# Second expert layer in pairs of 256 tokens, its first product as three fp32r products

## The reference, cut to what matters

```python
logits = x @ w_gate                      # 512 x 8
e_idx = np.argmax(logits, axis=1)        # one expert for each token
gate_w = softmax(logits)[arange, e_idx]
eom = 1.0 / (1.0 + np.exp(-(x @ w_output_gate)))
for e in range(8):
    mask = e_idx == e
    h = np.maximum(x[mask] @ w1[e], 0.0)             # 512 x 1024
    out[mask] = gate_w[mask] * eom[mask, e] * (h @ w2[e])   # 1024 x 512
```

## Time and profile before

| | |
|---|---|
| median of 3 runs | 690.13 us (688.09 to 690.76) |
| profiled execution, device time | 688.13 us |
| its span | 686.4 us |
| PE busy | 658.4 us, 96% |
| DVE, ACT, POOL busy | 60%, 49%, 43% |
| mean granted TensorE clock | 0.998 |

### The profile page before, as it was taken

One profiled execution on the slowest core, in us unless ns is written; L12 is line 12 of the kernel. 1 busy time (PEld: TensorE's weight loads), 2 busy tenths in 40 slices (PEclk: granted clock), 3 DMA queues, 4 the chain that ended last, 5 costly groups with the idle time before them and its releaser, 6 DMA issues.

```text
span 686.4 us, 15791 instructions
## 1 busy us (share of the span) xinstructions
PE 658.4 (96%) x5939; PEld 564.5 (82%) x5949; DVE 409.9 (60%) x859; ACT 337.0 (49%) x507; POOL 295.2 (43%) x287
## 2 busy tenths in 40 slices
PE   8989999999999989899999999989999999999995
PEld 5569889888888876479998998547999999999894
DVE  7878888788888857755454635375245254443421
ACT  4568999999999886331334312232213213231200
POOL 4357999989999871021221322002132132122121
PEclk9999999999999999999999999999999999999999
DMA  9301231111220439748489964654545654941000
GB/s 279 94 2 47 55 86 49 47 48 48 60 82 25 143 129 334 280 131 310 160 301 349 349 241 142 233 208 130 192 160 173 248 174 172 372 176 51 19 31 32
DMA packets 45988, 105.77 MB, mean 154 GB/s; under 512 B 5459, under 2 KB 11603, under 8 KB 45936
## 3 DMA queue, kind: packets, MB, share of 16 engines
q1 hardware_dynamic: 38464, 87.65, 36.8%
q0 software_dynamic: 4544, 12.70, 5.8%
q10 hardware_dynamic: 2928, 4.72, 2.0%
HBM read 87.64 MB, written 13.11 MB: 147 GB/s over the span
## 4 chain that ended last, share of the span: by engine, by line
PE 53%; DVE 3%; DMA 2%; issue 1%; ACT 0%; POOL 0%; POOLq 0%; ACTq 0%; DVEq 0%
PE hT_ps_layer L1381 27%; PE y_ps_layer L1394 7%; PE y_ps_layer L1398 7%; PE y_ps_layer L1401 7%; PE x_turn_layer L1368 2%; DMA x<-x_mid 1%; PE hT_ps_layer L1310 1%; PE hT_ps_layer L1308 1%; PE x_turn_layer L1298 1%; DVE row_one_hot_layer L1210 1%; DMA x_tile_layer<-x_src,token_to_read_layer 1%; PE hT_ps_layer L1323 1%; DMA x_mid<-y_out_layer,y_token_layer 0%; PE count_ps_layer L1298 0%; PE rank_ps_layer L1298 0%
## 5 line engine op out<-in xcount | busy, mean ns | idle before, releaser
L1381 PEld LDWEIGHTS hT_ps_layer<-xT_layer,w 128*128 128x128 f32 x1664 | 189.6, 192 | 3.8 <-DVE xT_layer L1243 1.7
L1381 PE MATMUL hT_ps_layer<-xT_layer,w 128*128 128x128 f32 x1664 | 190.2, 275 | 0.8 <-issue 0.8
L438 POOL TENSOR_TENSOR probs_lo<-probs,probs_hi 128x768 f16<-128x768 f32 x89 | 146.1, 1649 | 33.0 <-ACT probs_hi L353 30.4
L1132 ACT ACTIVATE hT_hi_layer<-hT_ps_layer 128x512 fp32r<-128x512 f32 x52 | 31.1, 597 | 239.2 <-PE hT_ps_layer L1381 239.2
L565 DVE TENSOR_REDUCE max_halves<-turn 128x1 f32<-128x384 f32 x180 | 94.7, 553 | 31.8 <-PE turn L729 30.2
L1270 DVE SCALAR_TENSOR_TENSOR hT_lo_layer<-hT_ps_layer,hT_hi_layer 128x512 fp32r<-128x512 f32 x52 | 34.6, 689 | 88.0 <-ACT hT_hi_layer L1132 77.0
L345 ACT ACTIVATE probs<-scores 128x768 f32<-128x768 f32 x96 | 79.9, 832 | 11.3 <-PE scores L753 10.3
L1445 POOL DMA_INDIRECT out_dram<-y_out_layer,y_token_layer x16 | 19.7, 1234 | 147.1 <-DVE y_out_layer L1281 147.1
L353 ACT ACTIVATE probs_hi<-scores 128x768 f16<-128x768 f32 x96 | 80.2, 836 | 1.2 <-PE pv L777 0.9
L1127 ACT ACTIVATE w_hi<-w 128x1024 fp32r<-128x1024 f32 x64 | 62.4, 1047 | 26.6 <-issue 26.6
L1250 DVE TENSOR_TENSOR w_lo<-w,w_hi 128x1024 fp32r<-128x1024 f32 x64 | 74.0, 1219 | 0.0
(11 more groups left out here) (227 smaller groups left out, 1087.5 us busy)
## 6 DMA issues: line engine op xcount, KB each, us to landing
w<-in_moe_w_dram SPq DMA_DIRECT2D x32, 2048.0 KB, 11.2
w<-in_v_dram ACTq DMA_DIRECT2D x4, 768.0 KB, 7.1
qk_raw<-in_q_dram SPq DMA_DIRECT2D x16, 192.0 KB, 3.2
qk_raw<-in_k_dram SPq DMA_DIRECT2D x16, 192.0 KB, 3.5
qB<-qA SPq DMA_DIRECT2D x16, 192.0 KB, 2.7
kB<-kA SPq DMA_DIRECT2D x16, 192.0 KB, 3.1
x_src<-x SPq DMA_DIRECT2D x2, 1536.0 KB, 17.0
x_mid<-x SPq DMA_DIRECT2D x2, 1536.0 KB, 18.3
```

The lines of the kernel that those rows point to most:

```text
L438: nc.gpsimd.tensor_tensor(p_lo[slot][:], probs[slot][:], p_hi[slot][:], ALU.subtract).then_inc(p_lo_pool, 1)
L1381: t = nc.tensor.matmul(hp[n][:, i * P:(i + 1) * P], W1[par][:, c, f * P:(f + 1) * P], xT[:, c, :], start=(c == 0), stop=(c == CD - 1))
```

## The change

In the second layer only:

- A step is a pair of tiles, 256 tokens of one expert. The table counts pairs; `read_tok` and the like have 30 columns instead of 24. An expert's last pair may be half or nearly empty, and is computed in full.
- The first product is three fp32r products of 256 moving columns: W1H x xTH, W1H x xTL, W1L x xTH. W1H and W1L lie in one buffer each (the place of `W2H[1]` and of the old `W2L`), so W2H has one buffer now and W2L a new one. DVE makes W1H by a copy and W1L by a subtraction, after the last pair of the expert before; for the first expert ACT and DVE make them at the end of layer one.
- x is gathered straight into the buffer that PE turns, two gathers for a pair; the `stage` copies and `turn_in` go. ACT takes the high part of the turned x, DVE the low part.
- ACT makes the output from PSUM (there are two banks for it), with the gate as a scale; DVE no longer does.
- The first product has four PSUM banks of two chunks each.

`w1_split(e)` is what DVE does after the last pair of expert e, for expert e + 1. The core of the diff, engine by engine:

```diff
         @blk.tensor
-            turn_x(0)
-            warm(5)
...
+            def turn_pair(g):
+                pe.wait_ge(x_in, 32 * g + 32)
+                for c in range(CD):
+                    for u in range(2):
+                        at = (c % 2) * R + u * P
+                        t = nc.tensor.transpose(tp[c // 2][:, at:at + P], xin[:, u, c * P:(c + 1) * P], ident[:])
+                    if c % 2 == 1:
+                        t.then_inc(x_turned, 1)
+
+            def pair_body(g, pair, par):
+                e = 2 * pair + par
+                pe.wait_ge(x_lo, 2 * g + 2)
+                for f in range(CF):
+                    b, i = divmod(f, 2)
+                    if i == 0:
+                        pe.wait_ge(w1_lo, W1_STEPS * e + f * W1_STEPS // CF + 1)
+                    h_ps = hp4[b][:, i * R:(i + 1) * R]
+                    at = slice(f * P, (f + 1) * P)
+                    for c in range(CD):
+                        nc.tensor.matmul(h_ps, W1H[:, c, at], xTH[:, c, :], start=(c == 0), stop=False)
+                        nc.tensor.matmul(h_ps, W1H[:, c, at], xTL[:, c, :], start=False, stop=False)
+                        t = nc.tensor.matmul(h_ps, W1L[:, c, at], xTH[:, c, :], start=False, stop=(c == CD - 1))
+                    if i == 1:
+                        t.then_inc(h_bank, 1)
+                turn_pair(g + 1)
+                for u in range(2):
+                    pe.wait_ge(y_ready, 2 * g + u + 1)
+                    at = slice(u * P, (u + 1) * P)
+                    for b in range(4):
+                        if u == 0:
+                            pe.wait_ge(h_hi, 4 * g + b + 1)
+                        for f in (2 * b, 2 * b + 1):
+                            nc.tensor.matmul(yp2[u][:], hH[:, f, at], W2H[par][:, f, :], start=(f == 0), stop=False)
+                        if u == 0:
+                            pe.wait_ge(w2_lo, W2_STEPS * e + b + 1)
...
+                    t.then_inc(y_done, 1)
...
         @blk.scalar
+            def x_to_hi(g):
+                for b in range(2):
+                    act.wait_ge(x_turned, 2 * g + b + 1)
+                    nc.scalar.activation(xTH[:, 2 * b:2 * b + 2, :].rearrange("p c n -> p (c n)"), tp[b][:], ACT.Copy).then_inc(x_hi, 1)
+
+            def pair_body(g, pair, par):
+                for b in range(4):
+                    act.wait_ge(h_bank, 4 * g + b + 1)
+                    nc.scalar.activation(hH[:, 2 * b:2 * b + 2, :].rearrange("p c n -> p (c n)"), hp4[b][:], ACT.Relu).then_inc(h_hi, 1)
+                x_to_hi(g + 1)
+                act.wait_ge(y_free, g + 1)
+                for u in range(2):
+                    act.wait_ge(y_done, 2 * g + u + 1)
+                    nc.scalar.activation(yout[:, u, :], yp2[u][:], ACT.Copy, scale=gate_col[:, u:u + 1]).then_inc(y_ready, 1)
...
         @blk.vector
+            def pair_body(g, pair, par):
+                for b in range(4):
+                    dve.wait_ge(h_hi, 4 * g + b + 1)
...
+                x_to_lo(g + 1)
...
+            def w1_split(e, pair, par):
+                if isinstance(e, int) and e == E - 1:
+                    return
+                dve.wait_ge(w1_ready[1 - par], 16 * (pair + par + 1 + E // 2))
+                for i in range(W1_STEPS):
+                    c = slice(i * F // W1_STEPS, (i + 1) * F // W1_STEPS)
+                    nc.vector.tensor_copy(W1H[:, :, c], W1[1 - par][:, :, c]).then_inc(w1_hi, 1)
+                    if i > 0:
+                        w1_rest(e + 1, 1 - par, i - 1)
+                w1_rest(e + 1, 1 - par, W1_STEPS - 1)
+                w1_taken(e + 1)
+                split(e + 1, None, 1 - par)
...
         @blk.gpsimd
+            def pair_body(g, pair, par):
+                pool.wait_ge(x_turned, 2 * g + 4)
+                nc.gpsimd.tensor_copy(gid[:], cols_of(read_tok, 2 * g + 4)).then_inc(gid_ready, 1)
...
+                gather_pair(gid)
+                pool.wait_ge(y_sent, 32 * g + 16)
+                nc.gpsimd.tensor_copy(gate_col[:], cols_of(gate_of, 2 * g)).then_inc(y_free, 1)
...
         @blk.scalar
...
             if first:
+                act.wait_ge(w1_ready[0], 16 * (1 + E // 2))
+                act.wait_ge(weights_over, 1)
+                for i in range(W1_STEPS - 1):
+                    c = slice(i * F // W1_STEPS, (i + 1) * F // W1_STEPS)
+                    nc.scalar.activation(W1H[:, :, c], W1[0][:, :, c], ACT.Copy).then_inc(w1_hi, 1)
```

## The result

Five runs of the changed kernel have a median of 693.57 us (692.69 to 694.40), five of the kernel before 690.56 (688.09 to 690.76): 1.0054 times as long, 95% interval 1.0035 to 1.0072. The medians lie 3.0 us apart, and the interval of the ratio is 2.4 to 5.0 us slower. The profiled execution took 692.69 us with a span of 691.0; before it was 688.13 and 686.4.

What follows compares the result with a forecast made beforehand. PE's own work was taken as the bound. 3.7 + 2.8 - 0.15 gave +6.3 us on the 686.4 span: 692.7, or 694.4 for the device; counted from 689.1, 695.5 us. Range: 686 to 703.

Steps and rivals of the forecast that it cites:

- the nine pairs: Layer two's loop on PE: nine pairs of 23.65 us, 212.9 against 209.2 for sixteen tiles, +3.7 us.
- between the layers: End of layer one: making expert 0's W1H and W1L there costed at nothing, up to 1 us if layer two starts late.
- a spacing below 119.4 ns: First-product matmul starts: 122 to 123 ns apart expected; below 119.4 the time is within 0.5%, below 111.3 faster.
- 15.9 ns over the columns: First product: surplus for each fp32r matmul, taken from the second product, giving 122.6 ns each, 11.77 us a pair.
- the surplus stands once for each matmul: fp32r matmuls: time over columns / 2.4 does not grow with the columns; 15 to 22 ns in the readings used.
- Rivals 1 and 2: First product 111.6 or 108.4 ns a matmul, 686 or 683, chance 0.19; surplus 4.9 in both products, 681, chance 0.08.
- rival 3: First product: weight load shows; with a 98 ns floor, 130 to 135 ns a matmul, 702 to 706, chance 0.12.
- The padding: Nine pairs compute 18 tiles where 16 were computed; y of the padding, 5.5 us a tile, twice, eats the gain.
- Start of the layer: Layer two's first product waits for two gathers and two more operations, 472.3 instead of 469.50: +2.8 us.
- The end: Last output of layer two moves from DVE's 0.76 us to ACT's 0.60: -0.15 us.
- DVE, ACT, POOL, SP behind PE: Other engines in layer two's pairs: their work is covered by PE's products, so PE does not wait; no cost.
- The room in the chain: DVE's preparation of weights in layer two: decisive only once 7 us later than reckoned; as a rival, chance 0.06.

Runs made afterwards that it cites:

- experiment 1: Changed kernel plus 216 matmuls before layer two's first product, a sweep of streams from 64 to 512 columns; 730.60 us in one run.
- experiment 4: Changed kernel with PE skipping, by a branch, 22 of 24 second-product matmuls of each empty tile; 686.31 us, 0.9931 times the kernel before.
- experiment 8: Changed kernel, first pair gathering only its first tile, turned twice: 693.91 us, 1.0052 times the kernel before; with warm matmuls moved and added, 692.85 us.
- experiment 3: Changed kernel without the product of low W1 and high x, 64 first-product matmuls a pair in place of 96; 664.03 us in one run.
- the repeat: The changed kernel measured once more, unaltered, beside later variants; 695.23 us, 1.0069 times the kernel before.

## Why the prediction was right

Slower, and PE as the bound of the loop with no wait in it, came out as forecast. What makes the kernel slower did not: the larger part of the forecast, 3.7 of 6.3 us, lay in the nine pairs, and they come out even (+0.3). That 693.57 lies near 695.5 is in part luck, since a loss between the layers that was costed at nothing covers part of that error. By the prediction's own sign, a spacing below 119.4 ns, the time should have been within 0.5% of before; at 118.3 ns it stands just past that edge (1.0054), because of the same loss. By its own terms:

- **The nine pairs, +3.7 us forecast, +0.3 measured.** This is the term that was mis-sized, at the step that took 15.9 ns over the columns from the second product. Measured are 11.6 at 256 columns: 4.3 ns x 864 = 3.7 us too much. y was 230.4 ns a matmul instead of 229.2, half a microsecond the other way. That the surplus stands once for each matmul, whatever the width, was wrong; it is smaller for narrow streams (experiment 1). Rivals 1 and 2 are refuted as they were sized: the surplus is neither 4.9 nor 1.7 ns, and in y it did not fall. But 512 columns of fp32r take 229.2 ns in y before, 230.4 after, 233 in the sweep and 235 in layer one, so something besides the width moves it; what, is open. The 98 ns that rival 3 read as a floor is one short stream of six; the other in attention (151.91 to 152.58) takes 112 ns a matmul, as the sweep does.
- **The padding.** What it costs was rightly seen: the two empty tiles cost 5.07 us each in y (experiment 4), a pair in place of two tiles gains 26.16 - 23.29 = 2.87 us, and the sixteen tiles need nine pairs, not eight.
- **Start of the layer, +2.8 forecast, +2.75 measured,** and for the reasons given (experiment 8).
- **Between the layers, nothing in the sum and up to 1 allowed, +1.4 measured.** I looked at whether DVE ends in time, not at what works beside it. It does end in time (436.71, the block change at 437.4), but the last send is 0.8 us longer beside it, and the loads of x take 0.9 us more.
- **The end, -0.15 forecast, +0.1 measured.** ACT's output takes 0.69 us, not 0.60. Up to the start of the last send the end is 0.24 us shorter, 685.15 - 683.14 against 680.90 - 678.65; from there to the end of the span it is 0.35 longer, and why is open.
- **DVE, ACT, POOL, SP behind PE: nothing forecast, nothing measured.** DVE's copy of 1024 columns took 0.69 us, the lower end of my 0.7 to 1.2. The room in the chain is about 3 us, less than I reckoned (experiment 3).

The sum was 6.3 us, the spans differ by 4.6, the medians by 3.0 here and by 6.1 in the repeat. Both first profiles are executions with the full clock in attention, so their 4.6 us compare like with like. The medians mix executions whose part ahead of the last send differs by up to 3.6 us with that clock, in the profiles at hand; whether the change has a hand in how often it falls there is not shown.

What the change hoped for, a cheaper first product, is there: 2.87 us for each two tiles. It is spent on two tiles of padding (their first product too, 5.7 us each), 2.75 us of start and 1.4 us between the layers. The skip gives back nearly half of the padding and ends ahead of both kernels: 685.4 to 686.3 us.

## What to carry to other kernels

Before widening a tile, count the tiles that the data makes: here 16 became 18. Eight pairs would have gained 23 us in the loop (8 x 2.87, an estimate); nine gave +0.3. Where a consumer throws a tile away, a branch round its matmuls cost 0.01 us a step. When work is moved into a quiet place, look at what runs there on the other engines: DVE's subtractions of two SBUF inputs beside a POOL send lengthened the send, and that was on the path. And before a difference of a few us is read from two profiles, compare the clock in the stages that the change does not touch.

## What the runs showed of the hardware

- In streams of 24 fp32r matmuls, each with its own 128 x 128 weights, one followed another in 110.4 ns at 64 and 128 columns and 110.8 at 192; from 256 columns on it took 7 to 11% over its columns: 118.3 ns at 256, 146.7 at 320, 173.3 at 384, 229 to 235 at 512.
- A plain fp32 matmul is two instructions of two passes each: 111.6 ns an instruction at 128 columns, 215.8 at 256, where two passes of the columns at 2.4 GHz are 106.7 and 213.3, so that at equal columns fp32 costs 3.65 times one fp32r matmul (2 x 215.8 / 118.3), and three fp32r products are 18% cheaper.
- An indirect DMA takes POOL 1.03 us, and 1.83 with DVE subtractions of two SBUF operands beside it. In layer one of the kernel before, seven of ten sends took 1.8 us, each with a W2 split of DVE beside it, and three 1.03 or 1.04, with none.
- The granted clock between 43 and 52 us was 1.00, 0.81 or 0.62 from one execution to another of the same code, and what follows came 1.4 to 3.6 us later when it was below 1.00.
